# Turning the activations on TensorE instead of VectorE in the last stage of an attention, expert and feed-forward kernel

## The reference

```python
def _moe2_ref(x, w_in, w_out, alpha) -> np.ndarray:   # x: rows of 512, w_in (512, 2048), w_out (2048, 512)
    h = x @ w_in
    g = np.maximum(h, 0.0) + alpha * np.minimum(h, 0.0)
    return (g @ w_out).astype(np.float32)
```

## Time and profile before

| what | value |
|---|---|
| median of three executions | 1458.1 us |
| the profiled execution's own time | 1459.01 us |
| its span in the profile | 1457.3 us |
| mean granted TensorE clock | 0.972 of full speed |
| TensorE matmul busy | 94% |
| VectorE, ScalarE, GpSimd busy | 45%, 27%, 13% |

### The profile page before, as it was taken

How to read it: one execution, slowest core, us unless ns; L and a number is a source line. 1 busy time by engine, 2 the same in 40 slices (tenths; PEclk the granted TensorE clock), 3 DMA queues, 4 the chain that set the end, 5 groups by cost and what they waited for, 6 DMA issues and landing times.

```text
span 1457.3 us, 18935 instructions
## 1 busy us (share of the span) xinstructions
PE 1363.7 (94%) x6716; PEld 1117.9 (77%) x6717; DVE 662.2 (45%) x953; ACT 399.9 (27%) x634; POOL 191.9 (13%) x235
## 2 busy tenths in 40 slices
PE   4998469999979999994999999999999999999998
PEld 4877358888868888883787878878788787887887
DVE  3677644222545435255554344354444534444343
ACT  5887312111333323134122121121211212112121
POOL 4564122111222222121000000000000000000000
PEclk9999669999989999997999999999999999999999
DMA  7785234111425224143201001010100101001000
GB/s 269 260 265 180 65 134 139 37 43 43 159 94 209 101 99 134 62 158 116 72 0 58 0 22 35 0 58 0 43 14 0 58 0 53 4 0 58 0 30 15
DMA packets 71483, 112.58 MB, mean 77 GB/s; under 512 B 6816, under 2 KB 38560, under 8 KB 70816
## 3 DMA queue, kind: packets, MB, share of 16 engines
q1 hardware_dynamic: 64192, 91.79, 18.7%
q0 software_dynamic: 6112, 19.93, 4.0%
q10 hardware_dynamic: 1152, 0.52, 0.1%
HBM read 84.17 MB, written 27.53 MB: 77 GB/s over the span
## 4 chain that ended last, share of the span: by engine, by line
PE 85%; DVE 5%; ACT 3%; DMA 2%; issue 2%; SPq 2%; POOL 0%; ACTq 0%; DVEq 0%; POOLq 0%
PE ps L316 9%; PE ps L318 9%; PE ps L317 9%; PE ps_o L318 7%; PE ps_o L316 7%; PE ps_o L317 7%; PE ps_h L316 5%; PE ps_h L318 5%; PE ps_h L317 5%; PE ps_y L316 5%; PE ps_y L318 5%; PE ps_y L317 5%; PE ps_hT L1209 2%; SPq L427 2%; PE ps_sr L1118 1%
## 5 line engine op out<-in xcount | busy, mean ns | idle before, releaser
L316 PE MATMUL ps<-yT_hi,w_hi 128*128 128x512 f32 (+1 forms) x576 | 221.9, 385 | 23.4 <-DVE yT_lo L1020 23.4
L751 ACT ACTIVATE gT_hi<-act_g 128x512 fp32r<-128x512 f32 (+1 forms) x144 | 87.7, 609 | 563.6 <-DVE act_g L1033 563.6
L1030 DVE TENSOR_SCALAR neg<-ps,alpha 128x512 f32<-128x512 f32 (+1 forms) x144 | 103.8, 721 | 293.0 <-PE ps L318 293.0
L318 PE MATMUL ps<-yT_hi,w_lo 128*128 128x512 f32 (+1 forms) x576 | 220.9, 384 | 0.0
L317 PE MATMUL ps<-yT_lo,w_hi 128*128 128x512 f32 (+1 forms) x576 | 220.8, 383 | 0.0
L318 PE MATMUL ps_o<-w_hi,gT_lo 128*128 128x512 f32 x544 | 212.2, 390 | 0.0
L316 PE MATMUL ps_o<-w_hi,gT_hi 128*128 128x512 f32 x544 | 211.9, 390 | 0.0
L317 PE MATMUL ps_o<-w_lo,gT_hi 128*128 128x512 f32 x544 | 211.8, 389 | 0.0
L316 PEld LDWEIGHTS ps<-yT_hi,w_hi 128*128 128x128 f32 x576 | 108.6, 189 | 49.6 <-DVE yT_lo L1020 26.5
L1036 DVE TENSOR_TENSOR gT_lo<-act_g,gT_hi 128x512 fp32r<-128x512 f32 (+1 forms) x144 | 95.4, 663 | 97.2 <-ACT gT_hi L751 97.2
L316 PE MATMUL ps_h<-w_hi,xgT_hi 128*128 128x512 f32 x296 | 122.8, 415 | 9.2 <-DVE w_lo L782 7.7
(11 more groups left out here) (177 smaller groups left out, 1739.1 us busy)
## 6 DMA issues: line engine op xcount, KB each, us to landing
stage<-in_moe_w SPq DMA_DIRECT2D x32, 1024.0 KB, 5.2
xs_all<-in_xT SPq DMA_DIRECT2D x8, 1024.0 KB, 6.6
xN_all<-in_xN SPq DMA_DIRECT2D x8, 1024.0 KB, 6.1
rows_x<-xrow SPq DMA_DIRECT2D x32, 256.0 KB, 2.5
yg<-rows_y SPq DMA_DIRECT2D x128, 64.0 KB, 1.9
out_rows<-orow SPq DMA_DIRECT2D x32, 256.0 KB, 2.0
stage<-in_moe_w_in SPq DMA_DIRECT2D x4, 1024.0 KB, 4.8
stage<-in_moe_w_out SPq DMA_DIRECT2D x4, 1024.0 KB, 5.6
```

Source lines behind the costliest of these rows:

```text
L316: pe.matmul(out, s_hi, m_hi, start=start, stop=False)
L318: return pe.matmul(out, s_lo, m_hi, start=False, stop=stop)
L751: act.activation(gT_hi[:, c % 2, f, 0:w], act_g[:, 0:w], ACT.Copy).then_inc(g_hi_ready, 1)
L1030: dve.tensor_scalar(neg[:, 0:w], ps_1[f][:, 0:w], 0.0, alpha[:, ft:ft + 1], ALU.min, ALU.mult)\
```

## The change

The 128x128 transposes are done by TensorE, four for a tile, with `ident` as the second operand and the result in PSUM (`ps_yT`, two new banks, so that all eight are in use). `yT` in SBUF and VectorE's `turn_y` are gone; the high and the low part are made from PSUM. A tile is loaded with one DMA of 256 KB in rows of 2 KB instead of four of 64 KB in pieces of 512 bytes; the first group's tiles 2 and 3 are loaded by SP too, and ScalarE loads none. The rows of `w_in` keep their order. The tiles after `yg` in SBUF move by the size of `yT`, 4 KB a partition. ScalarE's wait for the last up projection ahead of `y_hi` is gone. TensorE turns the next group's tiles 0 and 1 ahead of the last down projection (down(7)) and the tiles 2 and 3 in its middle.

TensorE at the end of a group in the loop, before: `ps_o` is the result of the down projection, `ps` of the up projection, `yT_hi` and `w_hi` the high parts.

The diff, without the lines that only name the constants `Q` and `QB`:

```diff
@@ buffers
-        yg = sb("yg", [P, 2, QB, P], c=sd)
-        yT = sb("yT", [P, 2, KD, P], c=sd)
+        yg = sb("yg", [P, 2, DM], c=sd)
         ps_1 = [pb(f"ps_1{i}", [P, 4 * P], c=pd) for i in range(FC)]
+        ps_yT = [pb(f"ps_yT{i}", [P, KD, P], c=pd) for i in range(2)]
@@ SP
-                rows = rows_y[bass.ds(t * P, P), :].rearrange("(j b) c -> b j c", j=QB)
-                for i in range(QB):
-                    sp.dma_start(yg[i * Q:(i + 1) * Q, k % 2, :, :], rows[:, :, i * P:(i + 1) * P])\
-                      .then_inc(y_loaded[k % 2], 16)
+                sp.dma_start(yg[:, k % 2, :], rows_y[bass.ds(t * P, P), :]).then_inc(y_loaded[k % 2], 16)
...
             for k in range(2):
                 load_tile(k, k, None)
+            for k in range(2):
+                sp.dma_start(orow[:, k, :], rows_y[(2 + k) * P:(3 + k) * P, :]).then_inc(y_early[k], 16)
@@ ScalarE
-            total = act.value_load(table[0:1, 3, E - 1:E], min_val=1, max_val=SLOTS)
-            wait_apart(act, scattered, 16 * total)
-            for k in range(2):
-                rows = rows_y[(2 + k) * P:(3 + k) * P, :].rearrange("(j b) c -> b j c", j=QB)
-                for i in range(QB):
-                    act.dma_start(orow[i * Q:(i + 1) * Q, k, :].rearrange("b (j c) -> b j c", j=QB),
-                                  rows[:, :, i * P:(i + 1) * P]).then_inc(y_early[k], 16)
...
-                act.activation(yT_hi[:, :, k * P:(k + 1) * P], yT[:, k % 2, :, :], ACT.Copy).then_inc(yT_hi_ready, 1)
+                act.activation(yT_hi[:, :, k * P:(k + 1) * P], ps_yT[k % 2][:], ACT.Copy).then_inc(yT_hi_ready, 1)
...
-                if nxt:
-                    act.wait_ge(p1_ready, g * KFF + KFF)
@@ VectorE
-            def turn_y(t, k, use):
...
-                dve.transpose(yT[:, k % 2, :, :].rearrange("p q (j b) -> p j q b", j=QB), src).then_inc(yT_ready, 1)
-
             def y_lo(t, k):
                 dve.wait_ge(yT_hi_ready, t + 1)
-                dve.tensor_tensor(yT_lo[:, :, k * P:(k + 1) * P], yT[:, k % 2, :, :],
+                dve.tensor_tensor(yT_lo[:, :, k * P:(k + 1) * P], ps_yT[k % 2][:],
...
                 for k in range(nxt):
-                    turn_y(4 * g + 4 + k, k, 2 * g + k // 2 + 2)
-                    if k:
-                        y_lo(4 * g + 3 + k, k - 1)
-                if nxt:
-                    y_lo(4 * g + 3 + nxt, nxt - 1)
+                    y_lo(4 * g + 4 + k, k)
@@ TensorE
+            def transpose_y(t, k, use):
+                if use is None:
+                    pe.wait_ge(y_early[k % 2], 16)
+                else:
+                    pe.wait_ge(y_loaded[k % 2], 16 * use)
+                if not (isinstance(use, int) and use == 1):
+                    pe.wait_ge(yT_lo_ready, t - 1)
+                src = orow if use is None else yg
+                for j in range(KD):
+                    mm = pe.transpose(ps_yT[k % 2][:, j, :], src[:, k % 2, j * P:(j + 1) * P], ident[:])
+                mm.then_inc(yT_ready, 1)
...
-                down(g, NC_ - 1, range(nt))
-
+
+                for k in range(0, nt, 2):
+                    for j in range(k, min(k + 2, nxt)):
+                        transpose_y(4 * g + 4 + j, j, 2 * g + j // 2 + 2)
+                    down(g, NC_ - 1, range(k, k + 2))
+
+            for k in range(4):
+                transpose_y(k, k, 1 if k < 2 else None)
             with pe.Fori(0, B - 1) as g:
-                group(g, 4)
-            group(B - 1, 4)
-            group(B, 2)
+                group(g, 4, 4)
+            group(B - 1, 4, 2)
+            group(B, 2, 0)
@@ host
-        "moe2_w_in": np.ascontiguousarray(moe2_w_in.reshape(QB, KD, Q, FF).transpose(1, 0, 2, 3)).reshape(DM, FF),
+        "moe2_w_in": np.ascontiguousarray(moe2_w_in),
```

More of the change, by code:

```diff
@@ L52 @@
 PB = 9
-Q = 32
-QB = P // Q
 TINY = 1e-30
@@ L1041, in group @@
                 for k in range(nxt):
-                    turn_y(4 * g + 4 + k, k, 2 * g + k // 2 + 2)
-                    if k:
-                        y_lo(4 * g + 3 + k, k - 1)
-                if nxt:
-                    y_lo(4 * g + 3 + nxt, nxt - 1)
+                    y_lo(4 * g + 4 + k, k)
             for k in range(4):
[L1049 to L1052, removed]
+                y_lo(k, k)
             group(0, 4, 4, rest_of_w_out=True)
@@ L1276, in down, with group @@
                         mm.then_inc(o_ready, 1)
-            def group(g, nt):
+            def group(g, nt, nxt):
                 w = nt * P
```

## The result

| kernel | median | executions |
|---|---|---|
| before | 1457.89 us | 4 (1457.24 to 1459.01) |
| after | 1466.60 us | 4 (1466.27 to 1467.40) |

The ratio is 1.0058, with a 95% interval of 1.0044 to 1.0073: the change costs 6.4 to 10.6 us. The forecast was 1460.7 us, +2.6, with a range from 1457.2 to 1465.2. The sign was right; the size was a third of the measured one, and the time lies above the range.

The account below looks back on a forecast made before the run. The prediction took TensorE, busy 94% of the span, to bound the kernel. Its terms, +11.8 - 5.15 - 4.7 + 0.65 = +2.6 us, gave 1460.7 us against the median of 1458.1, with a range from 1457.2 to 1465.2.

Parts of the forecast that it names:

- Sum: Whole kernel: the forecast's four terms added up to +2.6 us, giving 1460.7 us.
- the seven waits: Group boundaries of the last stage: TensorE's waits for the low part go, none for loads come; -5.15 us.
- the head: Start of the last stage: larger loads and a shorter chain let TensorE start at 688.15 instead of 692.89; -4.7 us.
- the clock: After the last stage's idle stretch: the clock's rise takes 3.1 to 6.0 us from the restart; +0.65 us.
- Transposes on TensorE: Dense work of the last stage: 15 pairs of tiles turned at 0.785 us a pair; +11.8 us.
- rival A: Group boundaries: loads of tiles 2 and 3 come late, up to +3.5 us; with a poor head 1466.4 us; 16%.
- Rival B: Last stage: up projection's matmuls take the down projection's faster pace, -10 us, 1451 us; 4%, its slower mirror image 3%.
- C: Start of the last stage: TensorE starts at 686.9 and a pair costs 0.70 us; 1457.4 us; 12%.
- D: Group boundaries: the 0.74 us gap is the loop's own edge and stays, so 1465.8 us; 3%.

Follow-up runs that it names:

- e10: The changed kernel run again with nothing altered: 1465.51 us, ratio 1.0057 to the kernel before.
- e1: The changed kernel with four load buffers instead of two: 1462.21 us, ratio 1.0035 to the kernel before.
- e9: The changed kernel with the second pair of transposes after 18 of the 24 matmuls instead of 12: 1465.41 us, ratio 1.0053 to the kernel before.
- e11: The changed kernel, two load buffers, with tiles 0 and 1 turned ahead of down(6), tiles 2 and 3 ahead of down(7): 1462.73 us, ratio 1.0037.
- e12: The changed kernel with four load buffers, run again beside the changed kernel on one chip: 1462.11 us, ratio 1.0035 to the kernel before.
- e2b: The changed kernel with four load buffers and one transpose of four for every tile of later groups: 1451.43 us, ratio 0.9963 to the kernel before.
- e2: The changed kernel, two load buffers, with one transpose of four for every tile of later groups: 1461.29 us, ratio 1.0027 to the kernel before.
- e4: The kernel before with four load buffers instead of two, nothing moved to TensorE: 1450.13 us, ratio 0.9956 to the kernel before.
- e8: The changed kernel with the first four tiles loaded by 16 DMAs of 64 KB on SP: 1466.80 us, ratio 1.0066 to the kernel before.

## Why the prediction failed, step by step

*Sum.* With the measured terms it is: clean pairs 15 x 0.877 = +13.2; late loads +3.6; the seven waits -5.8, by 7 x (89.19 - 88.36); the head -4.1; the clock +0.3. That is +7.2. With the late loads (+4.8) and the head (-3.8) of e10's profile it is +8.7. By medians it was +8.7 in the result and +7.9 in e10. Forecast: +11.8, 0, -5.15, -4.7, +0.65.

*Transposes on TensorE* was mis-sized, by 1.4 us, within its stated bounds. The 0.35 us for four in the earlier trace rows holds three steps of 0.11 and a short one of 0.03 to the matmul. By doubling it I counted the short step twice, but eight transposes in a row have it once: seven long steps and a short one are 0.79, and with the 0.09 behind them 0.88. e1, e9, e11 and e12 show 0.88 for every pair, and e2b gives the slope.

*The seven waits* is the step that failed. The low parts are in time, as it said. But "no wait, with 0.03 to 0.5 us to spare" for the loads took a landing of 2.0 to 2.5 us and 0.5 us between two issues. At the boundaries the loads of tiles 2 and 3 landed after 2.5 to 3.0 us, and the second went out 1.07 us after the first at one of them and 0.80 at six. TensorE lost 0.94 us at the first boundary and 0.21 to 0.64 at the others, 3.6 us in all (4.8 in e10), where the forecast had nothing. That is rival A, which I had given 16%. Its price for the loads, up to 3.5, was near; that its sum of 1466.4 meets the measured 1466.6 is luck, for it adds a poor head of 2.2 us that did not come and lacks what the pairs cost more. A margin smaller than the spread of the rows that it is made of should have been charged with part of its price in the forecast itself. And a nearer row was there for the step between two issues: in the trace of before, the 256 KB stores of the same loop go out 0.71 us apart. e1, e2, e11 and e12 show the late loads from four sides.

The gain of the same term was too small, by 0.65 us. A restart also costs in the matmul behind it, which the 5.15 leave out. At the first boundary of before (the line at 783.50 is in the earlier trace rows):

```profile
783.84 0.39 PE L317 MATMUL ps<-yT_lo,w_hi 128*128 128x512 f32 x1
```

This is 0.34 us behind the group's first matmul instead of 0.23, and so it is at all seven.

*The head* came out near: -4.1 for -4.7 in the two profiles of the result, less in most others. The chain of times (681.88 for the first transpose, 684.59 for the third tile, 687.94 for the first matmul, 8.70 us after the issue against the 8.05 of the forecast) has the shape of the forecast; tile 0 landed 0.5 later.

*The clock* was within its bounds (+0.3), in this execution.

*Rival B*, another pace of the matmuls, did not happen. The period of e1 less two pairs, 90.17 - 1.75 = 88.42 us, is within 0.06 us of e4's 88.36, which has the old code on TensorE. The up projection's pace is as before, 6 of them in 1.40 us (against the earlier trace rows):

```profile
782.12 0.40 PE L316 MATMUL ps<-yT_hi,w_lo 128*128 128x512 f32 x1
...
783.52 0.40 PE L316 MATMUL ps<-yT_hi,w_lo 128*128 128x512 f32 x1
```

*C* fell with the pair's price, *D* with e4. And one thing was missing from the whole argument: the wait that the change removed did not need it. In the kernel before it was a wait for loads too, at one remove. VectorE stood for tile 3's load just ahead of the parts that TensorE waited for:

```profile
781.34 0.71 DVE L1016 STREAM_TRANSPOSE yT<-yg 128x512 f32<-128x512 f32 x1 [0.82 <-DMA yg<-rows_y]
```

Two more load buffers end that wait (e4) with no work added to any engine.

## What to carry to other kernels

Before work is moved to the engine that bounds the kernel, see which wait the move is to end, and whether an earlier load ends it as well: here the kernel became 6.6 us faster without the move and 8 to 9 us slower with it. A margin between a load and its reader is to be held against the slowest landing and the slowest pitch of issues that any row shows, and what does not clear it is a part of the forecast. A run of small matmuls is to be priced by its number of steps, not by a shorter run doubled. A term read from one execution, such as the late loads here (3.6 and 4.8 us), is to be read from a second one before it is trusted to a microsecond.

## What the runs showed of the hardware

A second 256 KB load in SP's loop, issued with a register address behind a first, went out 1.07 us after it at the first boundary and 0.80 us after it at the other six, in the changed kernel and in e2, e9, e10 and e11 alike. In e8, with other code ahead of the same loop, it was 0.65 at all seven. The 64 KB loads of before go out 0.5 apart within a tile, and at the head two large ones with fixed addresses take 0.81 us together. Why these steps differ was not tried. The median read of 256 KB landed after 2.7 us where the writes of the same size took 2.0. TensorE's transposes of 128x128 float32 step by 0.109 us at full clock in every run where no wait stands between them. Behind a wait, the step from the group's first matmul to the second was 0.34 us instead of 0.23, at all seven boundaries of before and of e9. The granted clock rose between 3.07 and 5.75 us after the restart at the head of the last stage, in twelve profiles of kernels that are alike there in all but their loads and transposes.
